# Second-layer products and token mixing in halves of 256 columns

## What is computed

```python
def _moe_ref(x, w_tok1, w_tok2, w_ch1, w_ch2):
    xt = x.transpose(0, 2, 1)
    h = np.maximum(xt @ w_tok1, 0.0) @ w_tok2
    u = x + h.transpose(0, 2, 1)
    h2 = np.maximum(u @ w_ch1, 0.0) @ w_ch2
    return (u + h2).astype(np.float32)
...
def _moe2_ref(x, w_ch1, w_ch2):
    X = np.fft.fft(x, axis=1)
    X = np.fft.fft(X, axis=2)
    mixed = np.real(X).astype(np.float32)
    u = x + mixed
    mu = np.mean(u, axis=-1, keepdims=True)
    var = np.mean((u - mu) ** 2, axis=-1, keepdims=True)
    un = (u - mu) / np.sqrt(var + 1e-06)
    ch = np.maximum(un @ w_ch1, 0.0) @ w_ch2
    return (u + ch).astype(np.float32)
```

## Time and profile before

| | |
|---|---|
| median of 3 runs | 580.08 us (579.68 to 580.78) |
| the profiled execution's own time | 580.83 us |
| its span, first to last instruction | 579.0 us |
| instructions in the profile | 9534 |
| share of the span busy: TensorE, its weight loads | 98%, 87% |
| share of the span busy: VectorE, ScalarE, GpSimd | 62%, 44%, 42% |
| mean of HBM traffic | 84 GB/s |

### The profile page before, as it was taken

The page is one execution under the profiler, slowest core; times in us unless marked ns, Lnnn a source line. Parts: engine busy times, 40 slices in busy tenths (PEclk is TensorE's granted clock), DMA queues, the critical chain, the costliest instruction groups (busy, mean ns, idle before and its releaser), DMA issues.

```text
span 579.0 us, 9534 instructions
## 1 busy us (share of the span) xinstructions
PE 565.3 (98%) x3602; PEld 501.1 (87%) x3602; DVE 359.7 (62%) x634; ACT 253.2 (44%) x510; POOL 244.6 (42%) x241
## 2 busy tenths in 40 slices
PE   7999999999999999999989999999999999999997
PEld 6889887989898987899869978998888988989996
DVE  5676868676643895376969953769754643443333
ACT  2565434655544453334454533344453344344330
POOL 3342236366634453304767533047654333333311
PEclk9999999999999999999999999999999999999999
DMA  8980211422322120211112202111212122221142
GB/s 306 378 309 3 72 37 42 141 66 72 92 74 72 56 73 19 73 55 55 37 56 72 74 19 73 56 54 37 74 54 91 55 74 72 74 64 50 52 145 110
DMA packets 24157, 49.11 MB, mean 85 GB/s; under 512 B 2472, under 2 KB 3632, under 8 KB 24112
## 3 DMA queue, kind: packets, MB, share of 16 engines
q1 hardware_dynamic: 23520, 46.70, 23.8%
q0 software_dynamic: 448, 1.71, 1.0%
q10 hardware_dynamic: 144, 0.10, 0.1%
HBM read 45.35 MB, written 3.15 MB: 84 GB/s over the span
## 4 chain that ended last, share of the span: by engine, by line
PE 77%; DVE 16%; issue 3%; ACT 2%; DMA 1%; SPq 0%; DVEq 0%; ACTq 0%
PE banks L1095 12%; PE banks L1094 12%; PE banks L1093 12%; PE banks L1358 10%; PE banks L1360 9%; PE banks L1361 9%; DVE al L705 3%; PE banks L1172 2%; PE banks L1118 2%; PE banks L1181 2%; DVE u L875 2%; PE banks L1154 2%; DVE snap L992 1%; DVE h0l L778 1%; PE banks L1197 1%
## 5 line engine op out<-in xcount | busy, mean ns | idle before, releaser
L338 POOL TENSOR_TENSOR w2l<-raw,w2h 128x512 fp32r<-128x512 f32 x56 | 75.6, 1350 | 160.6 <-ACT w2h L453 160.6
L1358 PE MATMUL banks<-th,al 128*128 128x384 f32 x392 | 132.5, 338 | 1.2 <-DVE snap L992 0.4
L1360 PE MATMUL banks<-tl,ah 128*128 128x384 f32 x392 | 132.2, 337 | 0.0
L1361 PE MATMUL banks<-th,ah 128*128 128x384 f32 x392 | 132.0, 337 | 0.0
L453 ACT ACTIVATE snap<-banks 128x384 f32<-128x384 f32 x84 | 41.2, 491 | 137.0 <-PE banks L1361 129.8
L705 DVE TENSOR_TENSOR al<-raw,ah 128x512 fp32r<-128x512 f32 (+1 forms) x112 | 89.6, 820 | 5.0 <-ACT ah L453 3.9
L992 DVE TENSOR_TENSOR snap<-banks,snap 128x384 f32<-128x384 f32 x84 | 46.4, 552 | 65.9 <-PE banks L1361 65.5
L1358 PEld LDWEIGHTS banks<-th,al 128*128 128x128 f32 x392 | 73.6, 188 | 11.2 <-issue 3.1
L1360 PEld LDWEIGHTS banks<-tl,ah 128*128 128x128 f32 x392 | 73.5, 188 | 5.9
L1361 PEld LDWEIGHTS banks<-th,ah 128*128 128x128 f32 x392 | 73.6, 188 | 0.0
L338 POOL TENSOR_TENSOR raw<-raw 128x256 f32<-128x256 f32 x84 | 69.9, 848 | 2.2
(11 more groups left out here) (172 smaller groups left out, 890.6 us busy)
## 6 DMA issues: line engine op xcount, KB each, us to landing
raw<-w1b_dram SPq DMA_DIRECT2D x16, 512.0 KB, 3.2
raw<-w2b_dram SPq DMA_DIRECT2D x32, 256.0 KB, 3.0
raw<-w1a_dram SPq DMA_DIRECT2D x12, 512.0 KB, 3.2
raw<-w2a_dram SPq DMA_DIRECT2D x24, 256.0 KB, 3.2
kTs<-kT_dram SPq DMA_DIRECT2D x8, 384.0 KB, 6.0
qTs<-qT_dram SPq DMA_DIRECT2D x8, 384.0 KB, 7.0
kns<-kn_dram SPq DMA_DIRECT2D x8, 384.0 KB, 7.5
vns<-vn_dram SPq DMA_DIRECT2D x8, 384.0 KB, 5.4
```

The source lines that it names most:

```text
L338: return nc.gpsimd.tensor_tensor(o, i0, i1, ALU.subtract)
L1358: mm(o[:, 0:HALF], al[:, a, cols], th[b][:, t, k, :], start=start and k == 0, stop=False, skip_group_check=True)
L1360: mm(o[:, 0:HALF], ah[:, a, cols], tl[b][:, t, k, :], start=False, stop=False, skip_group_check=True)
L1361: last = mm(o[:, 0:HALF], ah[:, a, cols], th[b][:, t, k, :], start=False, stop=(k == 1), skip_group_check=True)
```

## The change

mm3_halves takes the place of mm3 in token_mix and in down. It does the three terms for columns 0 to 255 of the bank and then the three for columns 256 to 511. Each term is now two matmuls of 256 columns, each with its own load of the same weights. The flag that begins a new sum is set on the first matmul of the first half alone. The semaphore is raised by the last matmul of the second half, as before by the last of the three. All other users of mm3 (the Fourier stage) keep it.

```diff
+            def mm3_halves(o, lh, ll, rh_, rl_, start, stop):
+
+                for half in range(2):
+                    cols = slice(half * FH, (half + 1) * FH)
+                    mm(o[:, cols], ll, rh_[:, cols], start=start and half == 0, stop=False, skip_group_check=True)
+                    mm(o[:, cols], lh, rl_[:, cols], start=False, stop=False, skip_group_check=True)
+                    last = mm(o[:, cols], lh, rh_[:, cols], start=False, stop=stop, skip_group_check=True)
+                return last
...
-                    last = mm3(o, t2h[:, i, cols], t2l[:, i, cols], gh[:, KT * b + i, :], gl[:, KT * b + i, :],
+                    last = mm3_halves(o, t2h[:, i, cols], t2l[:, i, cols], gh[:, KT * b + i, :], gl[:, KT * b + i, :],
                                i == 0, i == KT - 1)
...
-                mm3(bank[t][:, :], hi, lo, w2h[:, i, :], w2l[:, i, :], j == 0 and i == 0,
-                    i == 1 and j == PAIRS[ch] - 1).then_inc(down_done, 1)
+                mm3_halves(bank[t][:, :], hi, lo, w2h[:, i, :], w2l[:, i, :], j == 0 and i == 0,
+                           i == 1 and j == PAIRS[ch] - 1).then_inc(down_done, 1)
```

## The result

The changed kernel took 586.12 us (median of 4 runs, 585.06 to 586.87), the kernel before 580.36 us beside it. The ratio is 1.0095, with an interval from 1.0081 to 1.0108: by that, 5.5 us more. The forecast was 577.8 us.

A forecast was written before the change was run, and what follows sets the result against it. TensorE's own time was taken as the bound. Run beginnings (-2.0) and products (-0.5), times 0.9, gave -2.3 us, from the median of 580.08 to 577.8 us; the range was 574.9 to 583.0 us.

The forecast's parts named there:

- What bounds the kernel: Whole kernel: TensorE, busy 98% of the span and 77% of the chain, so its savings are mostly saved at the end.
- Step 2: down and token_mix: 2160 added 256-column matmuls at 113.5 ns each, two costing 227.0 against 226.5; taken as 0, bound +0.5 us.
- The rule of the Trainium skill: Each matmul carries about 2.5 ns beside its columns, so 1080 more would cost 2.7 us; the forecast did not adopt it.
- Step 3: down and token_mix: 1080 more weight loads stay hidden at 256 columns, 109 ns shortest load distance against 113.5 ns.
- Step 4: Beginnings of the five down runs a pair get cheaper with halves: 0 to 2.5 us in all, 2.0 us taken.
- Step 5: 384-column products behind the runs may lose their excess of 0.07 us a pair: bounds 0 and -2.0 us, -0.5 taken.
- Step 6: Waits and queues: semaphores and other engines' work stay, waits take back some of the gain, so 0.9 of it is kept.
- Rival B: down and token_mix: short matmuls with a new moving operand each time take 119.1 ns per half, +8.3 us, 588.4 us; chance 0.10.

The follow-up runs named there:

- experiments 1 and 2: Streams of matmuls alone, one width and form each: halves settled at 120.0 ns; and the changed kernel with both halves of each term in succession: 585.66 us, ratio 1.0086.

## Why the prediction was wrong

- **What bounds the kernel** was right: TensorE's own pace was all that changed, and waits for VectorE hid it in the pairs that have them.
- **Step 2 failed, and with it the sign.** It priced a half at 113.5 ns from 23 rows of mix_half. Halves in down cost 120.0 settled and about 118 in short runs. The row was of the right width, with weights at another start modulo 128 bytes. It is not the rule for the operands of down: the two settled distances of streams whose starts agree, 173.3 ns at 384 columns and 226.5 at 512, lie on a line that gives 120.1 at 256, and streams alone gave 120.0. The prediction had both numbers and did not draw the line; instead it divided 226.5 by 512 for the price of a column, which hid a fixed part of 13 ns in it. The sum took 0 for this term; down's settled distances came to +0.48 us a pair. Even for mix_half 113.5 was the better of two paces, which two of eleven kernels showed.
- **The rule of the Trainium skill in step 2** ("TensorE: Matmul & The Clock Gate", section "Wait — 56ns, not 53.3ns?": a fixed cost of about 2.5 ns for each matmul) had the right form and direction, not the size. These runs have 13.3 ns in its place (226.7 - 512/2.4), for matmuls of the rounded format with a load each, and the measurement decides. Where the prediction said that the rows leave room for 0.5 ns, it used the wrong pair of rows.
- **Step 3** had the floor right (109 assumed from the transposes, 111 to 112 measured), and the loads ran beside the matmuls (PEld 95% busy). That loads play no part at 256 columns is not shown: 64 weight columns at 256 came at 113.3, but 32 at 117.7.
- **Step 4**, the beginning of a run, was right in direction and too small. Five runs of whole rows took 0.14 us more than their settled distances (226.7 ns), the five runs of halves 0.06 us less than theirs (72 x 120.0): 0.20 us a pair, where 0.07 was taken and 0.09 was the bound. The settled distances alone cost 72 x 120.0 - 36 x 226.7 = 0.48 us a pair. So a single down lost only 10 to 11 ns by the change, while six lost 186.
- **Step 5** was right in kind: products behind halves take 1.04 to 1.05 us for six instead of 1.06 or 1.07. It won 0.05 us a pair, near the upper bound of 0.07 where 0.02 was taken.
- **Step 6** was right in kind: where TensorE waits for VectorE the difference, here a loss, was absorbed. 28 undisturbed pairs would have lost 28 x 0.233 = 6.5 us; the span grew by 5.0.
- **Rival B** came true in its number (119.1 forecast, 118 to 120 measured) with a chance of 0.10, but not in its reason. The new moving operand each time costs nothing (experiments 1 and 2). Its price of +8.3 us was over the 5.5 measured, since it left out the products' gain and the pairs that wait. The argument against it was the row of mix_half again. Its signs came as named: six halves took 0.71 us, and TensorE's share of the chain rose.

The measured parts of the span: undisturbed pairs 13 x 0.233 = 3.0 us; the last pair with the down that follow it alone, 0.8 us (23.69 for 22.91); the fourteen other steps from pair to pair together 1.4 us; before the first product and behind the last matmul 0.26 us less. That makes the 5.0 us of the span.

## What to carry to other kernels

Price a narrower matmul from a line through two settled widths of streams with the same operands, not from the width alone. Here each matmul carried 13 ns beside its columns. Splitting 1080 of them would cost 1080 x 13.3 ns = 14.4 us by that alone; the beginnings of the runs, the products behind them and the waits left 5.0 us of it. Start addresses of weights and moving block are worth a look before any reordering: 64 bytes of padding were worth 4.2 us to the changed kernel and cost the kernel before 2.1 us (by the ratios 1.0095, 1.0023 and 1.0037).

## What the runs showed of the hardware that was not expected

- With a load of 128 weight columns for each matmul and starts that agree (modulo 128 or 256 bytes), streams in the rounded float32 format settle at 226.7, 180.0, 173.3, 146.7 and 120.0 ns for 512, 400, 384, 320 and 256 columns.
- With the weights 64 bytes off against the moving block: 233.3 ns at 512, 173.3 or 173.4 at 384, and 113.3 or 117.8 at 256, two settled paces of one stream.
- After a change of width the pace is unsettled for up to nine matmuls: in the kernel before the whole rows of the long run came at 229, 234, 235, 225, 230, 236, 229, 232 and 231 ns, then at 226 to 227. It depends on both widths: six products behind whole rows came at 168 to 185 ns each, behind halves at 172 to 178.
- A wait of 2.25 us inside the kernel was followed by a granted clock of 0.52 over 3.4 us, a wait of 0.85 us at the same place was not.

What stays open is the mechanism behind the offset and the two paces. It was shown that the distances follow the relative start, and that a pace can outlast a change of width, not why. What stays open too is where the 13 ns come from: they were measured, with a load in front of each matmul, and no run has the matmuls without loads. No version was found that is surely faster than the kernel before: the two nearest had ratios of 0.9991 (0.9981 to 1.0) and 0.9993 (0.9984 to 1.0002).
